# A feed-forward's second product turned round: token rows as the stationary operand

## The reference

```python
x  = attention(q, k, v, g_q, g_k)          # 4 x 12 heads, 448 tokens, 64 wide -> x [1792, 768]
e  = argmax(norm(x) @ norm(emb).T / tau)   # one of 8 experts for each token
p  = softmax(logits)[e]                    # its gate
y  = p * (relu(x @ w1[e]) @ w2[e])         # [1792, 768]
h  = y @ w_in                              # [1792, 2048]
g  = maximum(0.01 * h, h)
out = g @ w_out                            # [1792, 768]
```

## Time and profile before

| | us |
|---|---|
| median of 3 runs | 1249.09 (1248.95 to 1249.64) |
| the profiled execution | 1249.2 |
| span from its first to its last instruction | 1247.4 |
| PE busy in the span | 1196.3 (96%) |
| DVE, ACT, POOL busy | 873.2 (70%), 723.9 (58%), 604.3 (48%) |
| mean granted clock of PE | 0.985 of full |

### The profile page before, as it was taken

One profiled execution on the slowest core, in us unless ns is written; L12 is line 12 of the kernel. 1 busy time (PEld: TensorE's weight loads), 2 busy tenths in 40 slices (PEclk: granted clock), 3 DMA queues, 4 the chain that ended last, 5 costly groups with the idle time before them and its releaser, 6 DMA issues. The chain is left out here.

```text
span 1247.4 us, 21110 instructions
## 1 busy us (share of the span) xinstructions
PE 1196.3 (96%) x6978; PEld 1061.5 (85%) x6978; DVE 873.2 (70%) x1151; ACT 723.9 (58%) x1385; POOL 604.3 (48%) x655
## 2 busy tenths in 40 slices
PE   4999999999679999999999999999999999999995
PEld 3888888888568999999999988999999999999995
DVE  4999999999678999999999985455322255541222
ACT  4999999999646787887788763333311222211111
POOL 7898888887256767776776642221002001000012
PEclk9999999999869999999999999999999999999998
DMA  2244343322114554564454144441412212201221
GB/s 69 59 133 121 99 112 102 87 72 51 24 39 146 222 178 171 198 240 155 171 212 148 40 139 117 120 108 57 127 54 88 87 55 84 72 24 53 63 89 52
DMA packets 102426, 132.16 MB, mean 106 GB/s; under 512 B 32360, under 2 KB 81256, under 8 KB 102320
## 3 DMA queue, kind: packets, MB, share of 16 engines
q1 hardware_dynamic: 96048, 103.14, 26.7%
q0 software_dynamic: 6272, 27.68, 6.7%
HBM read 193.25 MB, written 19.34 MB: 170 GB/s over the span
## 5 line engine op out<-in xcount | busy, mean ns | idle before, releaser
L910 ACT CAST w_hi<-w_raw 128x768 fp32r<-128x768 f32 (+1 forms) x294 | 249.5, 930 | 16.7 <-DMA w_raw<-moe_w_in 11.1
L1104 DVE TENSOR_TENSOR w_lo<-w_raw,w_hi 128x1024 fp32r<-128x1024 f32 x82 | 181.3, 2246 | 1.3 <-ACT w_hi L910 1.3
L1436 POOL DMA_INDIRECT out_rows<-o_sb,out_index x23 | 22.2, 967 | 321.0 <-DVE o_sb L1583 320.7
L750 POOL TENSOR_TENSOR w_lo<-w_raw,w_hi 128x1024 fp32r<-128x1024 f32 x44 | 111.2, 2531 | 99.4 <-ACT w_hi L910 99.3
L1552 DVE TENSOR_TENSOR w_lo<-out_raw,w_hi 128x384 fp32r<-128x384 f32 x64 | 35.7, 558 | 166.7 <-ACT w_hi L1476 166.7
L1346 PE MATMUL ps_acc<-gT_hi,w_hi 128*128 128x448 f32 x384 | 141.7, 369 | 0.0
L1347 PE MATMUL ps_acc<-gT_hi,w_lo 128*128 128x448 f32 x384 | 139.7, 364 | 0.0
L1476 ACT CAST w_hi<-out_raw 128x384 fp32r<-128x384 f32 x64 | 32.8, 513 | 184.2 <-PE ps_acc L1348 184.0
L1348 PE MATMUL ps_acc<-gT_lo,w_hi 128*128 128x448 f32 x384 | 139.7, 364 | 0.0
L1112 DVE TENSOR_TENSOR w_lo<-w_raw,w_hi 128x768 fp32r<-128x768 f32 x126 | 138.7, 1163 | 0.0
L1470 ACT ACTIVATE small_h<-ps_acc 128x448 f32<-128x448 f32 x64 | 34.9, 545 | 168.7 <-PE ps_acc L1318 168.7
(11 more groups left out here) (224 smaller groups left out, 3135.9 us busy)
## 6 DMA issues: line engine op xcount, KB each, us to landing
w_raw<-moe_w_in SPq DMA_DIRECT2D x80, 1536.0 KB
in_raw<-moe_w_in_in SPq DMA_DIRECT2D x32, 384.0 KB, 4.1
out_raw<-moe_w_out_in SPq DMA_DIRECT2D x64, 192.0 KB, 2.3
qk_raw<-q_in SPq DMA_DIRECT2D x48, 112.0 KB, 2.0
qk_raw<-k_in SPq DMA_DIRECT2D x48, 112.0 KB, 2.2
v_raw<-v_in SPq DMA_DIRECT2D x48, 112.0 KB, 2.0
x_rows<-x_tok SPq DMA_DIRECT2D x48, 112.0 KB, 2.6
w_raw<-moe_w_in SPq DMA_DIRECT2D x6, 512.0 KB, 4.0
```

Of the source, the lines that this page charges most:

```text
L750: pool.tensor_tensor(w1_lo[:, c, :], w1_raw[:, c, :], w1_hi[:, c, :].bitcast(F32), ALU.subtract).then_inc(s_w1plo, 1)
L910: act.copy(out[:, c, :], raw[:, c, :]).then_inc(s_hi, 1)
L1104: dve.tensor_tensor(w1_lo[:, c, :], w1_raw[:, c, :], w1_hi[:, c, :].bitcast(F32), ALU.subtract).then_inc(s_w1lo, 1)
```

## The change

The second product's operands are exchanged. Stationary is a 128x128 piece of g (one inner chunk, one token tile), and w_out moves: 384 of its 768 columns at a time. The sums then have tokens on their partitions, and the transposes back fall away. The work is cut in 4 groups of token tiles, (0, 1, 2), (3 to 6), (7 to 10) and (11, 12, 13); a group of n tiles holds 2n banks and runs 16 steps of n x 2 x 3 matmuls, for which a 128x768 piece of w_out is loaded and split. The banks are one block of 8, used in pairs (`pair`). ACT and DVE copy one half of a tile each, with the gate as a factor, to one of three row buffers (`ring`, two of which are the shared `y_sb`); POOL scatters whole rows of 768 values, 14 times. The gathered rows of x use the same ring. The ids are used as they are, without the factor 2 for half rows. The places of `y_hi` and `y_low` in the loops change with the index of the steps. The diff, cut to its core:

```diff
-    K = C // 2
+    H = DM // 2
+    RING = 3
+    groups = ((0, 1, 2), (3, 4, 5, 6), (7, 8, 9, 10), (11, 12, 13))
+    pair = (2, 1, 0, 2, 1, 0, 3, 2, 3, 1, 0, 2, 3, 1)
+    hidden_before = {1: G - 2, 2: G - 1, 9: 2 * G - 2, 10: 2 * G - 1}
+    tile_before = {3: 0, 4: 1, 5: 2, 7: 3, 8: 6, 11: 7, 12: 8, 13: 9}
+
     with ExitStack() as ctx:
...
+        def hidden_bank(u, half):
+            return ps[:, 2 * (1 - u) + half, 0:Q]
+
+        def tile_bank(t, half):
+            return ps[:, 2 * pair[t] + half, 0:H]
+
+        y_banks = ps[:, 6:8, :]
 
...
+            def load_out(step, u):
                 if step > 1:
                     sp.wait_ge(s_outlo, step - 1)
-                sp.dma_start(out_raw[u][:, :], w_out[bass.ds(f * P, P), dh * K * P:(dh + 1) * K * P]).then_inc(s_out_in[u], 16)
+                f = step % G
...
+                if j < 2:
+                    sp.wait_ge(s_xss, J)
+                    sp.wait_ge(s_lg, J)
+                else:
                     sp.wait_ge(s_yt, j - 1)
...
+            for f in range(3, G):
+                load_in(f, f % 2)
+            for step in range(2 * G):
+                load_out(step, step % 2)
+                if 2 <= step < TILES + 2:
+                    load_y(step - 2)
+            for f in range(G):
+                load_in(G + f, f % 2)
+            for step in range(2 * G, 4 * G):
...
+            def output_step(g, f, u):
+                step = g * G + f
+                pe.wait_ge(s_outhi, step + 1)
+                pe.wait_ge(s_outlo, step + 1)
+                if g % 2 == 0:
+                    pe.wait_ge(s_ghi, G * (g // 2) + f + 1)
+                    pe.wait_ge(s_glo, G * (g // 2) + f + 1)
+                for t in groups[g]:
+                    rows = slice(t % TILES * P, (t % TILES + 1) * P)
                     for half in range(2):
-                        if first and n_pass % 2 == 0 and k < 2:
-                            pe.wait_ge(s_g, 2 * (G * (n_pass // 2 + 1) - 2 + k) + half + 1)
-                        elif first and n_pass > 0:
-                            pe.wait_ge(s_oT[half], K * (n_pass - 1) + order.index(k) + 1)
-                        cols = bass.ds(f * W + half * Q, Q)
-                        acc = ps_acc[:, 2 * k + half, 0:Q]
-                        hi, lo = (g[:, :, :].rearrange("p g w -> p (g w)")[:, cols] for g in (gT_hi, gT_lo))
-                        pe.matmul(acc, out_hi[u][:, k, :], hi, start=first, stop=False)
-                        pe.matmul(acc, out_lo[u][:, k, :], hi, start=False, stop=False)
-                        last = pe.matmul(acc, out_hi[u][:, k, :], lo, start=False, stop=final)
-                        if final and (k, half) != (order[-1], 1):
+                        if f == 0 and t in hidden_before:
+                            pe.wait_ge(s_g, 2 * hidden_before[t] + half + 1)
+                        if f == 0 and t in tile_before:
+                            pe.wait_ge(s_copied[half], tile_before[t] + 1)
+                        if f == 0 and t == TILES - 1:
+                            pe.wait_ge(s_yhi, TILES)
+                            pe.wait_ge(s_ylo, TILES)
+                        acc, cols = tile_bank(t, half), slice(half * C // 2, (half + 1) * C // 2)
+                        pe.matmul(acc, gT_hi[:, f, rows], out_hi[u][:, cols, :], start=f == 0, stop=False)
+                        pe.matmul(acc, gT_hi[:, f, rows], out_lo[u][:, cols, :], start=False, stop=False)
+                        last = pe.matmul(acc, gT_lo[:, f, rows], out_hi[u][:, cols, :], start=False, stop=f == G - 1)
+                        if f == G - 1 and (t, half) != (groups[g][-1], 1):
                             last.then_inc(s_full, 1)
...
+
+            for hf in range(2):
+                for f in range(G):
+                    if hf == 1 and f == 0:
+                        pe.wait_ge(s_yhi, TILES)
+                        pe.wait_ge(s_ylo, TILES)
+                    hidden_product(hf * G + f, f % 2)
+                for g in (2 * hf, 2 * hf + 1):
                     for f in range(G):
...
+                for g in (2 * hf, 2 * hf + 1):
-                    output_product(n_pass, f, f % 2)
-                    if 1 <= f <= TILES:
-                        if n_pass == 0:
+                        output_step(g, f, f % 2)
+                        if g == 0 and 1 <= f <= TILES:
                             transpose_y(f - 1)
-                        elif n_pass == 1:
...
+        def slot_free(engine, t):
+            if t >= RING:
+                engine.wait_ge(s_store[t % RING], 16 * (t // RING))
+            else:
+                engine.wait_ge(s_yt, TILES)
+                engine.wait_ge(s_gate, 1)
 
...
+            def store(t):
+                for half in range(2):
+                    pool.wait_ge(s_copied[half], t + 1)
+                pool.indirect_dma_start(out=out, out_offset=bass.IndirectOffsetOnAxis(ap=out_index[:, t:t + 1], axis=0),
+                                        in_=ring[t % RING][:, 0:DM], in_offset=None).then_inc(s_store[t % RING], 16)
...
+            def out_high(step, u):
+                act.wait_ge(s_out_in[u], (step - u) * 8 + 16)
+                if step > 1:
+                    act.wait_ge(s_used, step - 1)
+                act.copy(out_hi[u], out_raw[u][:, :, :]).then_inc(s_outhi, 1)
...
+            def copy_out(g, t):
+                full(act, g, t, 0)
+                slot_free(act, t)
+                act.activation(ring[t % RING][:, 0:H], tile_bank(t, 0), ACT.Copy, scale=gate[:, t:t + 1]).then_inc(s_copied[0], 1)
...
-                for dh in range(2):
-                    n_pass = 2 * hf + dh
-                    base = G * n_pass
-                    for f in range(2, G):
-                        out_high(f + base, f % 2)
-                        if n_pass == 0 and 3 <= f < TILES + 3:
-                            y_hi(f - 3)
-                        if n_pass == 0 and f == 4:
+                out_high(first + 1, 1)
+                for g in (2 * hf, 2 * hf + 1):
+                    for f in range(G - 1):
+                        step = g * G + f + 2
+                        if step < end:
+                            out_high(step, step % 2)
+                        if g == 0 and 2 <= f < TILES + 2:
+                            y_hi(f - 2)
+                        if g == 0 and f == 3:
                             exp()
-                    if dh == 0:
-                        out_high(base + G, 0)
-                    elif hf == 0:
+                    if g == 1:
                         in_high(G, 0)
                         in_high(G + 1, 1)
-                    for k in order:
-                        copy_acc(n_pass, k)
-                    if dh == 0:
-                        out_high(base + G + 1, 1)
+                    for t in groups[g]:
+                        copy_out(g, t)
+                    if g % 2 == 0:
+                        out_high(g * G + G + 1, 1)
+
         @block.vector
         def _(dve):
             def y_low(j):
...
+                for g in (2 * hf, 2 * hf + 1):
+                    for f in range(G - 1):
+                        step = g * G + f + 2
+                        if step < end:
+                            out_low(step, step % 2)
+                        if g == 0 and 2 <= f < TILES + 2:
+                            y_low(f - 2)
+                        if g == 0 and f == 1:
```

More of the change, by code:

```diff
@@ L1223, in feed_forward @@
         gT_hi, gT_lo = sb("gT_hi", [P, G, W], F32R), sb("gT_lo", [P, G, W], F32R)
[L1224 to L1229, removed]
+        out_raw = [sb(f"out_raw{u}", [P, C, P]) for u in range(2)]
@@ L1254, in stores_before @@
[L1254 to L1260, removed]
+        s_outhi, s_outlo, s_used, s_full = (sem(x) for x in ("s_outhi", "s_outlo", "s_used", "s_full"))
+        s_copied = [sem(f"s_copied{half}") for half in range(2)]
+        s_store = [sem(f"s_store{k}") for k in range(RING)]
+        in_cols = w_in.rearrange("(c p) f -> p c f", p=P)
+        steps = len(groups) * G
@@ L1306, in transpose_y @@
                 for c in range(C):
-                    last = pe.transpose(ps_tr[:, c // 3, (c % 3) * P:(c % 3 + 1) * P], y_g[j % 2][:, c * P:(c + 1) * P], consts["ident"][:, :])
+                    last = pe.transpose(y_banks[:, c // 3, (c % 3) * P:(c % 3 + 1) * P], y_g[j % 2][:, c * P:(c + 1) * P], consts["ident"][:, :])
                 last.then_inc(s_yt, 1)
[L1310 to L1319, removed]
             def hidden_product(hidden, u):
@@ L1353, in transpose_out @@
[L1353 to L1365, removed]
@@ L1388, in _ @@
-            for j in range(TILES):
-                transpose_out(3 * TILES + j)
-        def acc_ready(engine, n_pass, k, half):
-            if (k, half) == (order[-1], 1):
-                engine.wait_ge(s_acc, G * (n_pass + 1))
-            else:
-                engine.wait_ge(s_full, 5 * n_pass + 2 * order.index(k) + half + 1)
```

(54 more changed lines are left out.)

194 lines of the change are left out of this document (60 added, 134 removed).

## The result

The changed kernel takes 1260.06 us (median of 4 runs, 1259.0 to 1262.14), the kernel before 1249.06 (4 runs): ratio 1.0089, 95% interval 1.0072 to 1.0107. It is slower by 11.0 us where 13 were forecast. The profiled execution took 1260.9 us.

What follows compares the result with a forecast made beforehand. The prediction took PE, busy 96% of the span, as the bound up to the last matmul. Its terms, 2.7 - 6.9 - 6.9 + 18.8 + 1.0 + 0.9 + 3.4 = +13.0, on 1249.2 gave 1262.2 us, range 1253 to 1275.

Steps and rivals of the forecast that it cites:

- What bounds: Up to the last matmul, only changes to PE's own stream or waits imposed on PE move the time; PE 96% busy.
- Matmuls, +2.7: Second products: 1344 matmuls of 384 columns at 0.1755 us replace 1152 of 448 at 0.2024 us, +2.7 us.
- Transposes back, -6.9: 21 tiles' transposes back, in a pass or first product, go at 0.33 us each: -6.9 us.
- The end, -6.9: From last matmul to end of span: 9.1 us instead of 16.0, so -6.9 us.
- y, +18.8: Before transpose_y in the first part's second product, PE waits six times 3.14 us for y parts behind weight pieces: +18.8 us.
- First group's second step, +1.0: First part, first to second product: out_low(1) stands behind the last split_g, delaying step 1: +1.0 us.
- Ring, +0.9: Groups of four need a fourth slot: tile 10's copy waits for tile 7's scatter, delaying weight pieces: +0.9 us.
- Clock, +3.4: PE's clock falls to half level in two of the six y gaps, losing 1.7 us each: +3.4 us.
- case of up to three falls: The main forecast, with at most three clock falls in the y gaps: 1255 to 1267 us, chance 0.62.
- rival 1: The clock falls in every one of the six y gaps: 1269 us, or 1279 if it never rises between; chance 0.23.
- Rival 2: PE isn't held at transpose_y because the y parts are ready when it arrives: 1240 us; chance 0.10.
- Rival 3: Weight loads of 188 ns bound the 384-column matmuls: +16.8 us, 1279 us; chance 0.03.

Runs made afterwards that it cites:

- e4: e1 plus out_high(first + 1) and out_low(first + 1) ahead of the last scale_h and split_g, and g_sb as tile 10's row buffer: 1233.81 us, ratio 0.9881.
- e7: e4 with each row tile scattered as two half rows (28 scatters of 384 values) instead of one whole row: 1238.57 us, ratio 0.9915.
- e1: The changed kernel with y_hi and y_low called ahead of out_high and out_low on ACT and DVE: 1237.02 us, ratio 0.9908.
- e2: The kernel before the change with y_hi and y_low one turn later (f - 4 for f - 3): 1271.21 us, ratio 1.0166.
- e5: The changed kernel with only y_hi moved ahead of out_high, on ACT; DVE's order kept: 1259.94 us, ratio 1.0096.
- e6: The changed kernel with only y_low moved ahead of out_low, on DVE; ACT's order kept: 1257.09 us, ratio 1.0056.
- e3: The changed kernel with 24 unused 128-column matmuls ahead of the last six transposes of y, so PE works while waiting: 1257.36 us, ratio 1.0062.

## Why the prediction was right, point by point

- **What bounds.** Right: with the orders mended (e4), nothing but PE's stream sets the stage.
- **Matmuls, +2.7.** Right in kind, too large. The step that erred is the fixed part of a matmul, taken as 15.5 ns from the earlier trace rows. In e4's last product, which has no idle and a full clock, 671 spacings lie between 1106.81 and the last start at 1223.25: 173.5 ns, the quiet end of the earlier trace rows. 1344 x 0.1735 = 233.2 us, as before: 0. Why the second product had 15.7 ns beside the columns before, and has 13.5 now, stays open. The spacing also varies a little from step to step. In the timeline of the changed kernel, first and last of the 18 matmuls of step 0 (w_out parts in the shared `w1_hi`, `w1_lo`), then the last 13 of step 1 (in their own tensors):

```profile
868.26 0.34 PE L1345 MATMUL ps_f<-w_hi,gT_hi 128*128 128x384 f32 x1
...
871.23 0.34 PE L1347 MATMUL ps_f<-w_hi,gT_lo 128*128 128x384 f32 x1
...
873.37 0.33 PE L1347 MATMUL ps_f<-out_hi,gT_lo 128*128 128x384 f32 x1
...
875.45 0.34 PE L1347 MATMUL ps_f<-out_hi,gT_lo 128*128 128x384 f32 x1
```

174.7 ns (2.97/17) against 173.3 (2.08/12). The tensor isn't the cause of that difference: the steps alternate between the two places, and over e4's last product those from the shared tensors go every 173.3 ns, the others every 173.8.

- **Transposes back, -6.9.** Right: the second part's first product, with 7 of the 21 tiles, lost 2.3 us, 0.33 each as in the earlier trace rows.
- **The end, -6.9.** It was -8.2. Last matmul on PE; on DVE the gate copy of tile 11, the first of the last three; the first and the last of the three scatters; the landings:

```profile
1250.77 0.34 PE L1347 MATMUL ps_f<-out_hi,gT_lo 128*128 128x384 f32 x1
...
1249.06 0.62 DVE L1561 TENSOR_SCALAR y_sb<-ps_f,gate 128x384 f32<-128x384 f32 x1 [2.29 <-PE ps_f L1347]
...
1250.46 0.96 POOL L1414 DMA_INDIRECT out_rows<-y_sb,out_index  x1 [45.86 <-ACT o_sb L1473]
...
1252.99 0.96 POOL L1414 DMA_INDIRECT out_rows<-y_sb,out_index  x1 [0.30 <-issue]
```

```profile
DMA to landing us min/median/max: 3.0/3.0/6.3
```

The last scatter starts 1.9 us after the product's end (1251.11), not 1.3: the first one starts 1.40 us after its copy began, not the 0.89 of the earlier trace rows, and POOL's 1.26 us spacing hands that on. Why it is later isn't known; in e7, where the first scatter needs only ACT's half, it starts 0.85 us after that copy began (1223.08 to 1223.93). From its start to the end of the span it is 5.9 us, not 6.9 + 0.9: it does land 0.4 us later than the earlier trace rows, yet 1.0 us less follows its start than in the earlier trace rows. The number of buffers that POOL waits for at the end doesn't explain it: e4 and e7 both wait for four, and 5.8 us follow the last start in e4 (whole rows) and 6.5 in e7 (half rows). The tail goes with the half rows; its cause stays open.

- **y, +18.8.** The term that decides: six idles of 2.99 us, and 6.98 us from one `transpose_y` to the next at full clock, of which 3.14 are products and 0.65 transposes; 3.2 x 6 = 19.2. Shown from both sides, by taking the order away (e1), putting it into the kernel before (e2), and by each engine alone (e5, e6).
- **First group's second step, +1.0.** An idle of 0.86 and a late start of 1.0 between 871.23 and 872.42. Gone in e4.
- **Ring, +0.9.** 1.5, just above its upper bound of 1.4, and more in other profiled executions (2.1 in e3, 2.4 in e1). Tile 7's scatter, the copy of tile 10 that waits for its landing, and the matmul behind two roundings and remainders:

```profile
1198.38 0.96 POOL L1414 DMA_INDIRECT out_rows<-y_sb,out_index  x1 [178.56 <-ACT o_sb L1473]
...
1201.48 0.58 ACT L1473 ACTIVATE y_sb<-ps_f,gate 128x384 f32<-128x384 f32 x1 [3.10 <-DMA out_rows<-y_sb,out_index]
...
1203.92 0.42 PE L1345 MATMUL ps_f<-out_hi,gT_hi 128*128 128x384 f32 x1 [1.48 <-DVE out_lo L1528]
```

- **Clock, +3.4.** 5.95: four falls of 1.5 us each, not two of 1.7. The uncertainty had been named, the count was a guess. The profiled execution lies outside the case of up to three falls that got 0.62, and short of rival 1, which had a fall in every gap: the traces show 4, 5, 3 and 1 of six (changed, e2, e5, e6). The Trainium skill (page "TensorE: Matmul & The Clock Gate", section "HAM oscillation — how this bites in real kernels") tells of a loop with waits of about 3 to 5 us that falls in every iteration. The gaps here idle 2.5 to 3.0 us; the trace agrees in the kind of loss, and not in a fall each time.
- **Sum.** 0 - 6.9 - 8.2 + 19.2 + 1.0 + 1.5 + 6.0 = +12.6, and -1.4 from the spread before the stage: +11.2 of the 11.5 seen. The errors of 2.7 and 1.3 on one side and 2.6, 0.6 and 0.4 on the other nearly cancelled. The mechanism and its largest term were right; that the total came out within 2 us is in part luck.
- **Rival 2** (PE isn't held) fell at once; e1, 1237 us, is the kernel that it described at 1240. **Rival 3** (weight loads as the bound) fell too: weight loads are listed with a mean of 191 to 192 ns while the matmuls go every 173.5.

## What to carry to other kernels

When a loop's index is shifted, read for each engine's list what now stands ahead of the instruction that another engine waits for, and what event *that* one waits for: here a rounding for two steps later, bound to the end of the current step, took away a whole step of cover. Work that a neighbour waits for goes ahead of work for later, on every engine of the chain, since mending one of the two engines gave back 0 us (e5) and 3 us (e6), and mending both 23. And an idle of PE costs more than its length if it takes the clock with it: 18 us of waits cost 25, of which 6 are the clock.

## What the runs showed of the hardware that was not expected

- Six equal gaps (2.99 us idle, then 0.8 us of transposes, then 3.1 us of products) cost the clock in four cases; each time the half level (1.2 GHz) lasted 3.4 us, as in the earlier trace rows. At 2.8 us idle (e6) one of six fell in the profiled execution, but at 2.5 (e2) five of six, and in e3 a fall followed a single idle of 2.08 us. So in these traces the length of the idle alone doesn't tell whether the clock falls.
- 24 matmuls of 128 columns, each with its weight load, took 2.79 us (e3), at most 0.116 us each: with a third of the columns they are about two thirds as dear as one of 384 (0.1735), and they held the clock in all six gaps.
- An indirect scatter of 128 rows occupies POOL for 0.96 us and the next starts 1.26 us after it, for 1.5 KB rows (before, e7) as for 3 KB rows; the landing differs (medians 2.6 before and 3.0 after). So here the number of scatters weighs more at the end than their bytes: e7, with twice as many for the same bytes, ends 3.4 us later behind the last matmul.
